# Router scores of nine of twelve token tiles on VectorE instead of TensorE, in a two-layer mixture-of-experts kernel

## The chip, the cores and the metric

The kernel runs on one NeuronCore of a Trainium2 chip. The metric is the device time of one execution in microseconds (us), the median of several runs. The engines are named as in the profile: PE is TensorE, DVE is VectorE, ACT is ScalarE, POOL is GpSimd, SP only issues transfers.

## What is computed

The reference has three parts that follow one another. A recurrent attention over 2 batches, 8 heads and 768 steps gives x of shape (1536, 320). The first mixture (moe) sends every token through all four experts. The second (moe2) sends each token to the one expert with the highest score, out of eight, in slots of limited number:

```python
# first mixture, x: (1536, 320), w1: (4, 320, 1024), w2: (4, 1024, 320)
for e in range(4):
    h = np.maximum(x @ w1[e], 0.0)
    out += p[:, e:e + 1] * (h @ w2[e])
# second mixture, on that out: 8 experts, capacity 384
logits = x @ w_gate                      # w_gate: (320, 8)
expert_idx = np.argmax(logits, axis=1)
gate_w = softmax(logits)[arange(N), expert_idx]
# a token gets the next free slot of its expert; one that finds none is dropped
out[i] = gate_w[i] * y[expert_idx[i], pos[i]]
```

## The kernel before

The 1536 tokens are 12 tiles of 128 tokens, in 4 blocks of 3 tiles (`NT` = 3, `BLOCK` = 384, `BLOCKS1` = 4, `LAST1` = 3). A token's row of 320 features lies in one partition of `acc`, which sums the first mixture's output. Products are made in fp32r with each operand split into a high and a low part, and three products of parts stand for one.

**The loop over experts and blocks.** For each expert e of the first mixture and each block c, PE runs `up` (lines 516 to 531) and `down` (533 to 547). `up` makes 8 tiles of hidden features, f = 0 to 7, each out of 8 matmuls of 384 columns into one of three PSUM banks (`ps_h[f % 3]`). After each one ACT writes `h_hi` (`hidden_hi`, line 795) and then DVE `h_lo` (`hidden_lo`, line 1203). `up` waits ahead of tile f for `h_lo` of tile f - 3, since they share a bank. `down` makes the three token tiles n = 0, 1, 2, each out of 24 matmuls of 320 columns. Within n = 0 it waits ahead of each f for `h_lo` of that f. DVE then adds each tile into `acc` (`add_y`, line 1212). All of it is in program order on each engine. One block of one expert is called a block below, and T0 is the time of its first matmul.

**Weights.** Beside this the next expert's weights are prepared, one piece per block: ACT writes the high parts (`w_to_hi`, lines 787 and 790), DVE the tail (`w_tail`, line 1168, after `hidden_lo` of f = 3), and then POOL the low parts in two instructions (`w1_to_lo`, line 911, after `w_tail`, and `w2_to_lo`, line 919, after ACT's second). POOL's `w_to_lo` of moe2's first expert is needed only when moe2 begins.

**Routing.** The tokens' outputs are final in the last expert's blocks (e = 3). Their routing runs one block behind: in block c (1 to 3) the tiles of block c - 1 are routed, as group c - 1. The last block's tiles are routed as groups 3 (two tiles) and 4 (one tile), partly behind the loop. For a tile of an earlier block PE turns the 128x320 of `acc` with three transposes (`transpose_y`, line 587), ahead of f = 1, 2 and 3. ACT copies the result from PSUM into `yT` (lines 818 and 819), and PE multiplies it with the router's weights, three products of 8 columns (`logits`, line 598), ahead of f = 2, 3 and 4. DVE then chooses the expert (`choose_expert`, lines 1238 to 1253, ahead of and behind `hidden_lo` of f = 5), ACT takes the exponent behind its eight `hidden_hi` (line 824), and PE counts the earlier tokens of each expert (`count_earlier`, lines 603 to 615), ahead of `down`'s tile n = 1. DVE works out gates and slots behind `add_y` of n = 0 (`gates_of`, `slots_of`, lines 1256 to 1276). POOL scatters the group's rows into the table of slots (`scatter_rows`, line 1011) and doubles the last 64 features of each new tile (`repeat_tail`, line 1018).

**The chain on DVE.** Each routing instruction goes through `route`, which increments `route_step` and waits for it, so they follow one another without overlap. `count_earlier` waits for the fifth of a group (`CHOSEN`), and the scatter and the next group's `logits` for the fourteenth (`SLOTS`).

**The end of the loop.** Behind it come the last two groups, 34 products that keep PE busy while the table is read back, and the second mixture, expert by expert, with the same `up` and a `down` of its own (lines 660 to 704), `send` by POOL (line 1036) and w_tail with a share of w2's low part (line 1172).

Of the kernel before, what the change touches and what calls it, by code (L numbers as in the profile page):

```python
# [29 lines left out]
F32 = mybir.dt.float32  # L30
# [8 lines left out]
P = 128  # L39


def build_kernel(nc, gates, o_tok, qk_pair_t, q_t, kv_tok, probs, w_moe1, w_moe2, w_gate, out, capacity):
    BH, S = gates.shape[1:]
    CHUNKS = S // P
    HEADS, D = 8, q_t.shape[1] // 3
# [43 lines left out]
    LAST1 = BLOCKS1 - 1  # L89

    LAST_X = (1, 4)

    WARM_SHORT, WARM_GAP, WARM_LONG = 44, 14, 34

# [9 lines left out]
    with ExitStack() as ctx:  # L104
# [3 lines left out]
        def sem(name):  # L108
            return ctx.enter_context(nc.semaphore(name))
# [73 lines left out]
        w2_lo.append(sb("w2_lo_odd", [P, FT, X], F32R))  # L183
        small = ExitStack()
        empty_row = sb("empty_row", [P, ROW], F32, small)
        yT = [sb(f"yT{i}", [P, KT, P], F32, small) for i in range(NT)]
        top = sb("top", [P, NT], F32, small)
        shifted = sb("shifted", [P, NT, E2], F32, small)
# [105 lines left out]
        yt_psum = sem("yt_psum")  # L294
        yt_done = sem("yt_done")
        log_ready = sem("log_ready")
        route_step = sem("route_step")
        route_exp = sem("route_exp")
        count_ready = sem("count_ready")
# [14 lines left out]
        def _(sp):  # L314
# [48 lines left out]
            for p in range(PIECES):  # L363
                sp.wait_ge(w_ready, p + 1)
                load_piece(w_moe1, 1, p)

            sp.wait_ge(row_const, 1)
            sp.dma_start(table.rearrange("(n p) r -> p n r", p=P),
                         empty_row[:].unsqueeze(1).broadcast_to([P, E2 * NT, ROW])).then_inc(fill_done, 16)
            for par in range(2):  # L370
# [32 lines left out]
        def _(pe):  # L403
# [170 lines left out]
            def transpose_y(t):  # L574

                c, n = t // NT, t % NT
                pe.wait_ge(y_free, 3 + 3 * (G1 - BLOCKS1) + t + 1)
                if c < LAST1:

                    if t:  # L580
                        pe.wait_ge(yt_done, t)
                    dst = ps_yt[0]
                else:
                    dst = ps_yt[n]
                for k in range(KT):
                    width = P if k < 2 else TAIL
                    mm = pe.transpose(dst[0:width, k * P:(k + 1) * P], acc[:, t, k * P:k * P + width], ident[:])
                mm.then_inc(yt_psum, 1)

            def logits(t):  # L590
                for group in range(1, LAST1 + 1):
                    if t == GROUPS[group][0]:

                        pe.wait_ge(route_step, SLOTS * group)
                pe.wait_ge(yt_done, t + 1)
                for k in range(KT):
                    K = P if k < 2 else TAIL
                    mm = pe.matmul(ps_log(t, t + 1)[:, 0, :], yT[t % NT][0:K, k, :], wg[0:K, k, :],  # L598
                                   start=(k == 0), stop=(k == KT - 1))
                if any(t == tiles[-1] for tiles in GROUPS):  # L600
                    mm.then_inc(log_ready, 1)
# [16 lines left out]
            for c in range(BLOCKS1):  # L618
                def before_tile(f):
                    if f % 2 == 0:  # L620
                        pe.wait_ge(w_ready, 4 * e + f // 2 + 1)
                    if c and 2 <= f <= NT + 1:
                        logits(NT * (c - 1) + f - 2)
                    if c and 1 <= f <= NT:
                        transpose_y(NT * (c - 1) + f - 1)

                def before_products(n, f):
                    if c and n == 1 and f == 0:
                        count_earlier(c - 1)
                    if c == LAST1 and n == 2:  # L630
                        if f == 0:
                            transpose_y(TILES - 3)
                        if f == 2:
                            transpose_y(TILES - 2)
                        if f in (3, 4):
                            logits(TILES - 6 + f)
                up(BLOCKS1 * e + c, e % 2, lambda k: xt_hi[:, k, c * BLOCK:(c + 1) * BLOCK],
                   lambda k: xt_lo[:, k, c * BLOCK:(c + 1) * BLOCK], before_tile)
                down(BLOCKS1 * e + c, e % 2, before_products)
# [87 lines left out]
        def _(act):  # L727
# [85 lines left out]
            first_to_hi(3)  # L813

            def yt_to_sbuf(t):
                act.wait_ge(yt_psum, t + 1)
                src = ps_yt[t % NT if t // NT == LAST1 else 0]
                act.activation(yT[t % NT][:, 0:2, :], src[:, 0:2 * P].rearrange("p (k t) -> p k t", k=2), ACT.Copy)
                act.activation(yT[t % NT][0:TAIL, 2, :], src[0:TAIL, 2 * P:XD], ACT.Copy).then_inc(yt_done, 1)

# [20 lines left out]
            for c in range(BLOCKS1):  # L841
                for f in range(FT):
                    hidden_hi(BLOCKS1 * e + c, f)
                    if c and f < NT:
                        yt_to_sbuf(NT * (c - 1) + f)
                    if f in (3, 5):
                        w_to_hi(e + 1, (e + 1) % 2, c, f // 4)
                if c:
                    exp_logits(c - 1)
# [201 lines left out]
        def _(dve):  # L1051
# [184 lines left out]
            def choose_expert(group, part):  # L1236

                n = len(GROUPS[group])
                t = slice(GROUPS[group][0], GROUPS[group][0] + n)
                if part == 0:  # L1240
                    dve.wait_ge(log_ready, group + 1)
                    route(dve.tensor_reduce(top[:, 0:n], ps_log(t.start, t.stop), AX_X, ALU.max))

                    if group:
                        dve.wait_ge(route_exp, group)
                    route(dve.tensor_tensor(shifted[:, 0:n], ps_log(t.start, t.stop), over_e(top[:, 0:n]), ALU.subtract))
                    assert done[0] == SLOTS * group + SHIFTED
                else:
                    route(dve.scalar_tensor_tensor(cand[:, 0:n], shifted[:, 0:n], 0.0, below[:, 0:n],
                                                   ALU.is_equal, ALU.mult))  # L1250
                    route(dve.tensor_reduce(first[:, 0:n], cand[:, 0:n], AX_X, ALU.min))
                    route(dve.tensor_tensor(one_hot[:, t, :], below[:, 0:n], over_e(first[:, 0:n]), ALU.is_equal))
                    assert done[0] == SLOTS * group + CHOSEN
# [33 lines left out]
                return t.unsqueeze(2).broadcast_to([P, t.shape[1], E2])  # L1287


            dve.wait_ge(row_const, 4)  # L1290
            e = E1 - 1
            for c in range(BLOCKS1):
                g = BLOCKS1 * e + c
                for f in range(FT):
                    hidden_lo(g, f)
                    if f == 3:
                        w_tail(e + 1, (e + 1) % 2, c, slice(c * PF, (c + 1) * PF))
                    if c and f in (4, 5):
                        choose_expert(c - 1, f - 4)
                for n in range(NT):  # L1300
                    if c == LAST1 and n == 2:
                        choose_expert(LAST1, 0)
                        choose_expert(LAST1, 1)
                    add_y(g, NT * c + n, n, prob[:, NT * c + n, e:e + 1])
                    if c and n == 0:
                        gates_of(c - 1)
                        slots_of(c - 1)
            gates_of(LAST1)
# [113 lines left out]
```

## Time and profile before

| | us |
|---|---|
| median of 3 runs (each) | 612.3 (614.8, 607.52, 612.3) |
| the profiled execution's own time | 617.45 |
| its span, first to last instruction | 615.4 |
| PE busy | 586.8 |
| DVE busy | 286.2 |
| ACT busy | 217.0 |
| POOL busy | 202.7 |

The span is what the rows below count from; the execution's own time has 2.05 us around it. Busy time counts neither waits nor the issuing of transfers. The mean granted clock of PE over the span is 0.977 of full speed. The profile has several views: the page with its totals, groups of instructions by line, the timeline of one engine (each row: start in us, duration in us, engine, line, operation, output and inputs with shapes, count, and in brackets the idle time before it with what ended it), and windows, a table of each engine's busy time in stretches of time, with PE's granted clock.

### The profile page before, as it was taken

The numbers are of one execution on the slowest core, as the hardware profiler recorded it, in microseconds if no ns is written. First come the engines' busy times: TensorE is split into PE (matmuls) and PEld (weight loads), VectorE is DVE, ScalarE is ACT, GpSimd is POOL, SyncE is SP. The second block draws the span as 40 slices with busy tenths as digits, with TensorE's granted clock in tenths as the row PEclk, the third lists the DMA queues.
The fourth block names the chain that finished last, engine by engine and source line by source line (L and its number), as shares of the span: only waits on it lengthen the run. The fifth ranks groups of instructions, "written<-read, shape, count | busy, mean of one in ns | idle before, by whom it ended". The sixth has DMA issues, their size and how long they took to land.

```text
span 615.4 us, 10948 instructions
## 1 busy us (share of the span) xinstructions
PE 586.8 (95%) x4005; PEld 577.5 (94%) x4005; DVE 286.2 (47%) x597; ACT 217.0 (35%) x475; POOL 202.7 (33%) x226
## 2 busy tenths in 40 slices
PE   3989999999999999999999999999988998899996
PEld 3889989999999999999999999999978998899996
DVE  8577984322332332332233233342434499855472
ACT  5444573312321331232133123132205386546341
POOL 6445548101101110110111021312321567764461
PEclk9888999999999999999999999999987999899999
DMA  6674626931101101110110110211223657764400
GB/s 198 166 218 141 188 91 208 367 145 47 44 3 48 47 0 47 47 35 12 47 47 0 47 48 1 88 48 39 66 81 106 226 160 247 246 221 138 153 16 16
DMA packets 22428, 62.99 MB, mean 102 GB/s; under 512 B 3190, under 2 KB 12543, under 8 KB 22396
## 3 DMA queue, kind: packets, MB, share of 16 engines
q1 hardware_dynamic: 20476, 58.49, 29.5%
q0 software_dynamic: 1920, 4.07, 1.8%
q8 instruction: 21, 0.34, 0.2%
q14 instruction: 11, 0.09, 0.1%
HBM read 51.67 MB, written 13.11 MB: 105 GB/s over the span
## 4 chain that ended last, share of the span: by engine, by line
PE 84%; DVE 4%; DMA 4%; ACT 3%; issue 2%; POOL 1%; POOLq 0%; SPq 0%; DVEq 0%; ACTq 0%
PE bank L528 27%; PE bank L543 9%; PE bank L544 9%; PE bank L545 9%; PE bank L531 4%; PE bank L530 4%; PE bank L685 3%; PE bank L686 3%; PE bank L684 3%; PE bank L492 3%; PE bank L461 2%; DMA g_rows<-g_saved_rows 2%; PE bank L446 1%; PE bank L598 1%; PE bank L482 1%
## 5 line engine op out<-in xcount | busy, mean ns | idle before, releaser
L795 ACT ACTIVATE h_hi<-bank 128x384 fp32r<-128x384 f32 x192 | 94.7, 493 | 312.9 <-PE bank L531 312.8
L1203 DVE SCALAR_TENSOR_TENSOR h_lo<-bank,h_hi 128x384 fp32r<-128x384 f32 x192 | 105.6, 556 | 132.0 <-ACT h_hi L795 131.3
L911 POOL TENSOR_TENSOR w_lo_odd<-stage,w_hi_odd 128x512 fp32r<-128x512 f32 x24 | 31.3, 1303 | 149.2 <-DVE w_hi_odd L1168 119.7
L911 POOL TENSOR_TENSOR w_lo_even<-stage,w_hi_even 128x512 fp32r<-128x512 f32 x24 | 31.3, 1306 | 132.7 <-DVE w_hi_even L1168 119.6
L528 PE MATMUL bank<-xt_hi,w_hi_even 128*128 (+2 forms) x192 | 65.3, 340 | 3.8 <-DVE h_lo L1203 2.1
L528 PE MATMUL bank<-xt_hi,w_hi_odd 128*128 128x384 f32 (+2 forms) x192 | 63.6, 331 | 2.2 <-DVE h_lo L1203 2.2
L1212 DVE SCALAR_TENSOR_TENSOR acc<-bank,prob,acc 128x320 f32 (+1 forms) x36 | 19.8, 551 | 95.8 <-PE bank L545 95.8
L528 PE MATMUL bank<-xt_lo,w_hi_even 128*128 (+2 forms) x192 | 63.6, 331 | 0.0
L528 PE MATMUL bank<-xt_hi,w_lo_even 128*128 (+2 forms) x192 | 63.5, 331 | 0.0
L528 PE MATMUL bank<-xt_lo,w_hi_odd 128*128 128x384 f32 (+2 forms) x192 | 61.8, 322 | 0.0
L528 PE MATMUL bank<-xt_hi,w_lo_odd 128*128 128x384 f32 (+2 forms) x192 | 61.8, 322 | 0.0
L543 PE MATMUL bank<-w_hi_odd,h_hi 128*128 128x320 f32 x192 | 59.9, 312 | 0.0
L543 PE MATMUL bank<-w_hi_even,h_hi 128*128 128x320 f32 x192 | 59.4, 309 | 0.2 <-DVE h_lo L1203 0.2
L544 PE MATMUL bank<-w_lo_odd,h_hi 128*128 128x320 f32 x192 | 59.3, 309 | 0.0
L545 PE MATMUL bank<-w_hi_even,h_lo 128*128 128x320 f32 x192 | 59.3, 309 | 0.0
L545 PE MATMUL bank<-w_hi_odd,h_lo 128*128 128x320 f32 x192 | 59.3, 309 | 0.0
L544 PE MATMUL bank<-w_lo_even,h_hi 128*128 128x320 f32 x192 | 59.3, 309 | 0.0
L528 PEld LDWEIGHTS bank<-xt_hi,w_hi_even 128*128 128x128 f32 x192 | 36.8, 192 | 4.8 <-DVE h_lo L1203 2.6
L528 PEld LDWEIGHTS bank<-xt_hi,w_hi_odd 128*128 128x128 f32 x192 | 36.1, 188 | 2.8 <-DVE h_lo L1203 2.7
L528 PEld LDWEIGHTS bank<-xt_lo,w_hi_even 128*128 128x128 f32 x192 | 36.9, 192 | 0.0
L528 PEld LDWEIGHTS bank<-xt_hi,w_lo_even 128*128 128x128 f32 x192 | 36.7, 191 | 0.0
L755 ACT ACTIVATE dmat<-bank,cols 128x128 f32<-128x128 f32 x96 | 27.2, 366 | 27.0 <-PE bank L446 27.0
(183 smaller groups left out, 1348.4 us busy)
## 6 DMA issues: line engine op xcount, KB each, us to landing
stage<-w_moe SPq DMA_DIRECT2D x48, 704.0 KB, 4.1
slot_rows<-empty_row SPq DMA_DIRECT2D x1, 4632.0 KB, 20.1
x_slot<-slot_rows SPq DMA_DIRECT2D x24, 193.0 KB, 4.3
kv<-kv_tok SPq DMA_DIRECT2D x12, 324.0 KB
qk_pair<-qk_pair_t SPq DMA_DIRECT2D x24, 160.0 KB
q_rows<-q_t SPq DMA_DIRECT2D x12, 180.0 KB
sig<-o_tok SPq DMA_DIRECT2D x2, 960.0 KB, 6.5
out<-empty_row SPq DMA_DIRECT2D x2, 960.0 KB, 17.8
```

Of the source, the lines that this page charges most:

```text
L492: mm = pe.matmul(ps_in[:, h * V1:(h + 1) * V1], pmat[:, h, :], v41[j][:, h, :], start=True, stop=True)
L528: pe.matmul(dst, wk[w][:, k, cols], xk(k), start=(n == 0), stop=False)
L530: pe.matmul(dst, w1_hi[w][:, 2, cols], xh(2), start=False, stop=False)
L531: pe.matmul(dst, w1_hi[w][:, 2, cols], xl(2), start=False, stop=True).then_inc(h_psum, 1)
L543: pe.matmul(ps_y[n][:, 0:X], h_hi[:, f, rows], w2_hi[w][:, f, :], start=(f == 0), stop=False)
L544: pe.matmul(ps_y[n][:, 0:X], h_hi[:, f, rows], w2_lo[w][:, f, :], start=False, stop=False)
L545: mm = pe.matmul(ps_y[n][:, 0:X], h_lo[:, f, rows], w2_hi[w][:, f, :], start=False, stop=(f == FT - 1))
L755: op = act.activation(dmat[b][:, h, :], src[:, n * P:(n + 1) * P], ACT.Exp, bias=cols3[:, c, b * HEADS + h:b * HEADS + h + 1])
L795: act.activation(h_hi[:, f, :], ps_h[f % 3][:, 0:BLOCK], ACT.Relu).then_inc(h_hi_done, 1)
L911: return pool.tensor_tensor(w1_lo[w][:, :, cols], raw1[:, 0:2, :], w1_hi[w][:, 0:2, cols].bitcast(F32), ALU.subtract)
L1203: dve.scalar_tensor_tensor(h_lo[:, f, :], ps_h[f % 3][:, 0:BLOCK], 0.0, h_hi[:, f, :].bitcast(F32), ALU.max, ALU.subtract).then_inc(h_done, 1)
L1212: op = dve.scalar_tensor_tensor(acc[:, tile, 0:X], ps_y[n][:, 0:X], share, acc[:, tile, 0:X], ALU.mult, ALU.add)
```

## The change

The scores of groups 0 to 2 (nine tiles) are made on DVE. The router's weights come in a second array, `w_gate_rows` (8 x 320), which is sent to all 128 partitions with one broadcast transfer. One score of 128 tokens is one `scalar_tensor_tensor`, (acc * 1.0) * weights' row, with the sum in `accum_out`: 24 of them to a group. Two stand behind each `hidden_lo` of a block and eight behind the last one. Then comes `choose_expert`. PE's `transpose_y` and `logits` and ACT's copies of `yT` for these groups are left out, `count_earlier` moves from n = 1 to n = 2 of `down`, and gates and slots from behind `add_y` of n = 0 to behind that of n = 1. The tiles of the last block go as before.

```diff
+        wg_rows = sb("wg_rows", [P, E2, X], F32, small)
+        products = [sb(f"products{i}", [P, X], F32, small) for i in range(3)]
+        logit = sb("logit", [P, TILES - NT, E2], F32, small)
...
             sp.wait_ge(row_const, 1)
+            sp.dma_start(wg_rows[:], w_gate_rows.unsqueeze(0).broadcast_to([P, E2, X])).then_inc(wg_rows_in, 16)
             sp.dma_start(table.rearrange("(n p) r -> p n r", p=P),
...
                 def before_tile(f):
                     if f % 2 == 0:
                         pe.wait_ge(w_ready, 4 * e + f // 2 + 1)
-                    if c and 2 <= f <= NT + 1:
-                        logits(NT * (c - 1) + f - 2)
-                    if c and 1 <= f <= NT:
-                        transpose_y(NT * (c - 1) + f - 1)
 
                 def before_products(n, f):
-                    if c and n == 1 and f == 0:
+                    if c and n == 2 and f == 0:
                         count_earlier(c - 1)
...
                     hidden_hi(BLOCKS1 * e + c, f)
-                    if c and f < NT:
-                        yt_to_sbuf(NT * (c - 1) + f)
...
                 if part == 0:
-                    dve.wait_ge(log_ready, group + 1)
-                    route(dve.tensor_reduce(top[:, 0:n], ps_log(t.start, t.stop), AX_X, ALU.max))
+                    if group < LAST1:
+                        dve.wait_ge(dot_done, NT * E2 * (group + 1))
+                        log = logit[:, t, :]
+                    else:
+                        dve.wait_ge(log_ready, group - LAST1 + 1)
+                        log = ps_log(t.start, t.stop)
+                    route(dve.tensor_reduce(top[:, 0:n], log, AX_X, ALU.max))
...
+            def dots(group, part):
+                for n in range(DOTS * part, DOTS * (part + 1)):
+                    t = NT * group + n // E2
+                    if n % E2 == 0:
+                        dve.wait_ge(y_free, 3 + 3 * (G1 - BLOCKS1) + t + 1)
+                    k = NT * E2 * group + n
+                    if k >= 3:
+                        dve.wait_ge(dot_done, k - 2)
+                    dve.scalar_tensor_tensor(products[k % 3][:], acc[:, t, 0:X], 1.0, wg_rows[:, n % E2, :], ALU.mult, ALU.mult,
+                                             accum_out=logit[:, t, n % E2:n % E2 + 1]).then_inc(dot_done, 1)
...
             dve.wait_ge(row_const, 4)
+            dve.wait_ge(wg_rows_in, 16)
...
                     if f == 3:
                         w_tail(e + 1, (e + 1) % 2, c, slice(c * PF, (c + 1) * PF))
-                    if c and f in (4, 5):
-                        choose_expert(c - 1, f - 4)
+                    if c:
+                        dots(c - 1, f)
+                if c:
+                    for part in range(FT, NT * E2 // DOTS):
+                        dots(c - 1, part)
+                    choose_expert(c - 1, 0)
+                    choose_expert(c - 1, 1)
                 for n in range(NT):
                     if c == LAST1 and n == 2:
                         choose_expert(LAST1, 0)
                         choose_expert(LAST1, 1)
                     add_y(g, NT * c + n, n, prob[:, NT * c + n, e:e + 1])
-                    if c and n == 0:
+                    if c and n == 1:
                         gates_of(c - 1)
                         slots_of(c - 1)
```

`DOTS` is 2 and `E2` is 8. The new tiles lie in the memory that later holds the slots' rows.

## Rows read from the trace of the kernel before

**Rows 1.** The page, part 1: busy time, share of the span, instructions.

```profile
PE 586.8 (95%) x4005; PEld 577.5 (94%) x4005; DVE 286.2 (47%) x597; ACT 217.0 (35%) x475; POOL 202.7 (33%) x226
```

**Rows 2.** Windows, last expert's blocks 0 and 1: length, engines' busy, clock, DMA share, GB/s.

```profile
349.36:371.01 21.65, 21.65 (x139) 21.65 (x137) 6.53 (x12) 5.29 (x10) 3.35 (x4) 1.00 0.11 34
371.01:396.31 25.30, 25.30 (x168) 25.04 (x167) 9.81 (x26) 6.90 (x17) 6.23 (x6) 1.00 0.14 46
```

**Rows 3.** Timeline of PE, block 1 of the last expert.

```profile
371.01 0.33 PE L528 MATMUL bank<-xt_hi,w_hi_odd 128*128 128x384 f32 x1
...
374.12 0.82 PE L598 MATMUL bank<-wg,yT 128*128 128x8 f32 x6
...
381.42 0.34 PE L528 MATMUL bank<-xt_hi,w_hi_odd 128*128 128x384 f32 x1
...
385.58 0.31 PE L543 MATMUL bank<-w_hi_odd,h_hi 128*128 128x320 f32 x1
```

**Rows 4.** Timeline of DVE, the same block.

```profile
373.12 0.56 DVE L1203 SCALAR_TENSOR_TENSOR h_lo<-bank,h_hi 128x384 fp32r<-128x384 f32 x1 [1.35 <-ACT h_hi L795]
...
384.28 0.18 DVE L1251 TENSOR_REDUCE first<-cand 128x3 f32<-128x24 f32 x1
384.50 1.32 DVE L1252 TENSOR_TENSOR one_hot<-below,first 128x24 bf16<-128x24 f32 x1
385.85 1.02 DVE L1203 SCALAR_TENSOR_TENSOR h_lo<-bank,h_hi 128x384 fp32r<-128x384 f32 x2
```

**Rows 5.** Timeline of POOL, the same block.

```profile
381.13 1.29 POOL L911 TENSOR_TENSOR w_lo_even<-stage,w_hi_even 128x512 fp32r<-128x512 f32 x1 [9.07 <-DVE w_hi_even L1168]
384.20 1.57 POOL L919 TENSOR_TENSOR w_lo_even<-stage,w_hi_even 128x640 fp32r<-128x640 f32 x1 [1.78 <-ACT w_hi_even L790]
392.58 1.19 POOL L1011 DMA_INDIRECT slot_rows<-acc,slot  x1 [6.80 <-DVE slot L1275]
...
396.33 0.42 POOL L1018 COPY acc<-acc 128x64 f32<-128x64 f32 x2
```

**Rows 6.** Timeline of DVE, second mixture: operations on SBUF alone, and what follows them.

```profile
475.78 0.49 DVE L1172 TENSOR_TENSOR w_lo_odd<-stage,w_hi_odd 128x320 fp32r<-128x320 f32 x1
476.19 0.55 DVE L1203 SCALAR_TENSOR_TENSOR h_lo<-bank,h_hi 128x384 fp32r<-128x384 f32 x1
...
481.44 0.18 DVE L1334 COPY gate_s<-x_slot 128x3 f32<-128x3 f32 x1
481.54 0.15 DVE L1335 CAST token_s<-x_slot 128x3 uint32<-128x3 f32 x1
```

**Rows 7.** One line's instructions, durations in ns: minimum, median, maximum.

```profile
L1249 DVE SCALAR_TENSOR_TENSOR cand<-shifted,below x5: 167/173/175, 384.1 to 453.0; 128x24 f32<-128x24 f32 x3, 128x16 f32<-128x16 f32 x1, 128x8 f32<-128x8 f32 x1
```

**Rows 8.** Timeline of ACT, block 1 of the last expert.

```profile
383.39 0.73 ACT L790 ACTIVATE w_hi_even<-stage 128x640 fp32r<-128x640 f32 x1
```

**Rows 9.** Timelines of DVE, POOL and PE in the second mixture.

```profile
509.25 2.98 DVE L1172 TENSOR_TENSOR w_lo_odd<-stage,w_hi_odd 128x320 fp32r<-128x320 f32 x1
...
509.75 1.31 POOL L911 TENSOR_TENSOR w_lo_odd<-stage,w_hi_odd 128x512 fp32r<-128x512 f32 x1
511.00 0.87 POOL L919 TENSOR_TENSOR w_lo_odd<-stage,w_hi_odd 128x320 fp32r<-128x320 f32 x1
...
512.75 0.38 PE L528 MATMUL bank<-xt_hi,w_hi_even 128*128 128x256 f32 x1 [2.07 <-DVE h_lo L1203]
...
527.37 0.39 PE L528 MATMUL bank<-xt_hi,w_hi_odd 128*128 128x256 f32 x1 [2.18 <-DVE h_lo L1203]
```

**Rows 10.** Windows of 1 us behind the two gaps; the column before the last two is the clock.

```profile
514.00:515.00 1.00, 1.00 (x9) 1.00 (x8) 0.99 (x2) 1.00 (x3) 0.44 (x1) 1.00 0.89 366
...
529.00:530.00 1.00, 1.00 (x6) 1.00 (x5) 0.99 (x3) 1.00 (x3) 0.13 (x2) 0.50 0.77 321
...
532.00:533.00 1.00, 1.00 (x9) 1.00 (x8) 0.96 (x4) 0.00 (x0) 0.01 (x1) 0.96 0.28 93
```

**Rows 11.** The page, part 5: ACT's copies of the staged weights.

```profile
L787 ACT ACTIVATE w_hi_even<-stage 128x768 fp32r<-128x768 f32 x24 | 20.4, 849 | 0.0
```

More of the change, by code:

```diff
@@ L39, with build_kernel @@
 P = 128
-def build_kernel(nc, gates, o_tok, qk_pair_t, q_t, kv_tok, probs, w_moe1, w_moe2, w_gate, out, capacity):
+def build_kernel(nc, gates, o_tok, qk_pair_t, q_t, kv_tok, probs, w_moe1, w_moe2, w_gate, w_gate_rows, out, capacity):
     BH, S = gates.shape[1:]
@@ L91, in build_kernel @@
     LAST_X = (1, 4)
+    DOTS = 2
     WARM_SHORT, WARM_GAP, WARM_LONG = 44, 14, 34
@@ L296, in build_kernel @@
         log_ready = sem("log_ready")
+        wg_rows_in = sem("wg_rows_in")
+        dot_done = sem("dot_done")
         route_step = sem("route_step")
@@ L577, in transpose_y @@
                 pe.wait_ge(y_free, 3 + 3 * (G1 - BLOCKS1) + t + 1)
[L578 to L584, printed above, removed]
+                dst = ps_yt[n]
                 for k in range(KT):
@@ L590, in logits @@
             def logits(t):
[L591 to L595, printed above, removed]
+                if t == GROUPS[LAST1][0]:
+                    pe.wait_ge(route_step, SLOTS * LAST1)
+                pe.wait_ge(yt_done, t - NT * LAST1 + 1)
                 for k in range(KT):
@@ L815, in yt_to_sbuf @@
             def yt_to_sbuf(t):
-                act.wait_ge(yt_psum, t + 1)
-                src = ps_yt[t % NT if t // NT == LAST1 else 0]
+                act.wait_ge(yt_psum, t - NT * LAST1 + 1)
+                src = ps_yt[t % NT]
                 act.activation(yT[t % NT][:, 0:2, :], src[:, 0:2 * P].rearrange("p (k t) -> p k t", k=2), ACT.Copy)
@@ L1240, in choose_expert @@
                 if part == 0:
-                    dve.wait_ge(log_ready, group + 1)
-                    route(dve.tensor_reduce(top[:, 0:n], ps_log(t.start, t.stop), AX_X, ALU.max))
+                    if group < LAST1:
[5 more added lines that the diff above has]
+                    route(dve.tensor_reduce(top[:, 0:n], log, AX_X, ALU.max))
                     if group:
                         dve.wait_ge(route_exp, group)
-                    route(dve.tensor_tensor(shifted[:, 0:n], ps_log(t.start, t.stop), over_e(top[:, 0:n]), ALU.subtract))
+                    route(dve.tensor_tensor(shifted[:, 0:n], log, over_e(top[:, 0:n]), ALU.subtract))
                     assert done[0] == SLOTS * group + SHIFTED
@@ L1412 @@
         "w_gate": w_gate,
+        "w_gate_rows": inputs["moe2_w_gate"].T,
     }
```

## The prediction

> **What bounds the kernel now.** The page's totals come first: PE is busy 95% of the span, DVE 47% [rows 1]. The chain that ended last runs over PE's matmuls almost throughout, so time taken from PE's program counts in full, as long as its feeders keep pace. Next, the windows of the stretch in question: a block without routing takes 21.65 us and the next, with routing, 25.30 us, PE being busy throughout at full clock [rows 2]. DVE is busy 6.53 and 9.81 us in them, so it seems to have 15 us to spare. But the reader has to see when that time is free. DVE's h_lo is what PE waits for: PE's tile f needs h_lo of f - 3, and the product f of the first token tile needs h_lo of f. Work put between them is on the path once it outgrows its gap.
>
> **What goes.** Between T0 = 371.01 and 381.42 PE makes five hidden tiles, and three more up to 385.58, 1.387 us each [rows 3]. Five would take 6.93 us; they took 10.41. So nine transposes and eighteen small products cost 3.48 us a block, 10.4 us in three blocks. ACT's copies go too; ACT has room already, so this is worth nothing by itself. One group of each kind of row shows it: the products L598 at 374.12 stand between hidden tiles with nothing beside them [rows 3].
>
> **What one dot costs.** No row shows an instruction with `accum_out`. The nearest is DVE's 128x320 operation with two inputs in SBUF: 0.49 us long, the next one starting 0.41 us behind it [rows 6]. Then the sum has to be written. At best that is hidden: 0.41 us. At worst it waits for the end of the main part and takes a small chained routing operation's step, 0.22 us from 384.28 to 384.50 [rows 4]: 0.49 + 0.20 = 0.69. A small operation that waits for nothing costs 0.10 us (481.44 to 481.54) [rows 6]. I take 0.58, which is 0.49 and about that 0.10. It is nearest to what a second small instruction should cost behind one whose end it needs.
>
> The Trainium skill (VectorE: DVE Perf Modes, "Two Vector instructions with no wait between them") says that an operation which also writes its accumulator is two instructions. It gives no price; the ends above stand without it.
>
> A wait stands ahead of each dot, for the dot three before it. That has long ended, so it costs nothing. Behind it queue the next h_lo, and PE for that.
>
> **Where they fall: the up phase.** Times are from T0. The first h_lo starts at 2.11 and the spacing of two is 0.46 to 0.47 [rows 4]. ACT offers a new one each 1.387 us. An h_lo and two dots take 0.47 + 1.16 = 1.63, so DVE falls behind from the start: h_lo of f = 1, 2, 3 at 3.74, 5.37 and 7.00. w_tail then ends at about 8.0.
>
> Now a second thing. POOL makes its two low parts, 1.29 and 1.57 us [rows 5], and while it does so, DVE's operations with both inputs in SBUF stand. In this very block one_hot, a 0.17 us operation by its neighbours, starts at 384.50 and takes 1.32 us, to 385.82, just behind POOL's end at 384.20 + 1.57 = 385.77 [rows 4, 5]. A w2 part in the second mixture took 2.98 us in place of 0.49, over two POOL instructions that follow each other directly (509.75 to 511.87) [rows 9]. h_lo reads PSUM and SBUF and isn't held; a dot is. POOL starts as w_tail ends, one dot passes, and the second one stands. ACT's second part has ended by 9.7 (it is 0.73 us long and follows hidden tile 5) [rows 8], so POOL's second instruction follows the first at once, to about 11.35. That dot ends at 11.8, and h_lo of f = 4, queued behind it, at 12.4. PE needs it for tile 7, due at 9.71: a stall of 2.75 us. Tile 7 ends at 13.84. h_lo of 5, 6, 7 start at 13.43, 15.06, 16.69; the last ends at 17.25. PE wants it at 16.92, and 0.35 us more go. Tiles n = 0 and 1 of down end at 17.74 and 21.26 (3.52 each, from 10.56 us a down in the plain block [rows 2, 3]).
>
> **The down phase.** DVE has ten dots left from 17.16, so it is at 22.96. Then come the drain of the last (0.1) and five chained routing operations of 0.21: CHOSEN at 24.1. `count_earlier` waits for that, and PE's tile n = 2 is queued behind it: a wait of 2.85 us, though the change moved the count a whole tile later. Tile 2 ends at 27.8 (0.1 for the count, then 3.52). The block takes 27.8 us against 25.3: +2.5, or +7.5 for three. DVE then has its adds, gates and slots (13 short operations, some 3 us) done by 27, so nothing is carried over to the next T0.
>
> **Edges.** POOL's scatter starts some 5 us later in the block than now (21.6), at about 27, and takes 3.75 us up to the copies (392.58 to 396.33) [rows 5]. So three copies of 0.24 fall into the next block's first dots and hold them: 0.5 us, in two blocks, +1.0. In block 3 the transposes of the new tile wait for `add_y` behind CHOSEN (0.3), and its scores for the slots of group 2 at 27 (0.5): +0.8. The broadcast transfer of 1.3 MB on SP's queue stands ahead of the table's filling in the first expert. It delays the weights of the third by some us, but ACT's copies of them show no idle time at all ahead of them [rows 11], so it costs nothing.
>
> **The clock.** PE's waits of 2.85 us are new. The trace has two waits of nearly this size: behind one of 2.07 us the granted clock stayed at 1.00, the 2.4 GHz level; behind one of 2.18 us it fell to 0.50, the 1.2 GHz level, from 529 to just past 532 [rows 9, 10]. Three us at half speed cost 1.6. The new waits are longer than both. The wait in the up phase lies ahead of PE's longer wait in down, which absorbs a slower n = 0 and 1; the wait ahead of n = 2 isn't covered by anything. I count two falls of three: +3.2, with 0 and 4.8 as ends.
>
> **Sum.** 7.5 + 1.0 + 0.8 + 3.2 = 12.5 us. The profiled execution's own 617.45 becomes 629.95. It lies 5.15 over the median shown, 612.3, and on that scale the forecast is 624.8, slower by 2.0%.
>
> **Rivals.**
> 1. *The two sides cancel.* With a dot at 0.50 or less, each block is shorter by 24 x 0.08 = 1.9 us or more, which leaves +0.6 or less a block, and the waits of PE drop under 1.5 us, below the one that left the clock alone. With the edges the sum is between -1 and +4: 611 to 616. For it: the spacing of 0.41 [rows 6]. Against: the sum must be written. The bound to the forecast lies at 0.52.
> 2. *Faster.* POOL's lows hold no dot, and a dot takes 0.48 or less. Then h_lo of 7 ends by 12.7 (2.11 + 7 x 1.43 + 0.56), PE's up phase keeps its 11.1, and CHOSEN comes at 19.1, 1 us behind n = 1: the block takes 22.8, -2.5 each, 605. The decisive point is the hold; [rows 4, 5] and [rows 9] both speak for it, so this is unlikely.
> 3. *The dot runs at half rate.* 320 elements cost 0.33 us more, 0.91 in all; DVE bounds the block by 24 x 0.33 = 7.9 us more, +24 in three blocks: 648. Against it: the same kind of instruction with two SBUF inputs takes 0.167 us at 8 elements and 0.173 at 24 [rows 7]. At half rate 16 elements more should cost 0.033. These are short operations, though, and carry no sum.
>
> The Trainium skill (Vector Engine (DVE) Microarchitecture Reference, "Points that are easy to get wrong") says of this instruction that two SBUF sources which aren't bf16 halve its throughput, as no port is left for the accumulator. That is rival 3. By that rule the time would be the 648 above; the trace so far leans against it.
>
> **How the numbers follow.** About 1% (6 us) is what a measurement of this kernel can tell from no change. Chances: the forecast and its neighbourhood (dot 0.52 to 0.69) 0.54, rival 1 0.24, rival 2 0.10, rival 3 0.12. Faster by over 1%: 0.10. Within: 0.24. Slower: 0.66. The forecast's own range is from 618 (dot 0.52) to 0.11 x 24 x 3 = 8 us over it with a third fall of the clock, 635. With rival 1 at the lower end and something of a dearer dot at the upper one the range is 608 to 640; it leaves out most of rivals 2 and 3.
>
> **What would show it.** In the changed profile: dots of 0.49 us with a second small row or a gap behind each, spacing 0.58; in each of three blocks one dot of 2 us or more beside POOL's L911 and L919; PE waiting for h_lo at tile 7 and for one_hot ahead of n = 2, both 2 to 3 us; PE's rows L587 and L598 down to a quarter; windows of 27 to 29 us per block, some with the clock under 1.00. If those windows are under 25.3, DVE's slack was real and the forecast is wrong; if dots beside POOL keep their length, the hold is the step that failed; if the blocks exceed 33, it is the price of a dot.

## The result, and the profile after

The median of 20 runs is 609.4 us against 613.2 us of 20 runs before. The ratio is 0.9945, with a 95% interval of 0.9919 to 0.997: faster by 0.3 to 0.8%, some 2 to 5 us. Here and below, ratios and intervals leave out runs over 1.5% above the fastest of their kernel. The forecast was slower by 12.5 us, so the sign is wrong. The profiled execution has a span of 609.2 us against 615.4, but half of that difference means nothing for the change. Block 1 begins at 367.86 in place of 371.01 [rows 3], so 3.15 us were gained ahead of the altered blocks. That is how one execution differs from another: over the profiles of all runs below the same T0 lies anywhere from 364.2 to 375.7. The one thing altered ahead of it is the broadcast transfer, and ACT's first copies of the staged weights have one and the same wait for a transfer in both kernels, 2.6 us near 100 us (ahead of a copy into w_hi_odd, which the row of [rows 11] leaves out), so it cost nothing, as predicted. The blocks have to be compared from their own T0.

Windows of the changed kernel: the last expert's blocks 0, 1 and 3 (the columns are those of [rows 2]).

```profile
346.21:367.86 21.65, 21.65 (x139) 21.65 (x137) 6.54 (x12) 5.29 (x10) 3.35 (x4) 1.00 0.11 34
367.86:391.98 24.12, 22.51 (x142) 21.70 (x140) 20.84 (x74) 5.51 (x11) 3.45 (x4) 1.00 0.10 32
...
416.16:441.00 24.84, 23.06 (x151) 21.84 (x149) 20.85 (x74) 6.59 (x15) 7.37 (x9) 1.00 0.16 54
```

Block 0 is unaltered at 21.65. Block 1 takes 24.12 us in place of 25.30 [rows 2], block 2 24.18 in place of 25.39, and from the last T0 to the second mixture's first matmul it is 42.39 in place of 43.30. That is 1.18 + 1.21 + 0.91 = 3.3 us, close to the medians' 3.8. DVE is busy 20.84 of 24.12 us, where it was 9.81 of 25.30, and PE now has 1.6 us of idle time. The clock stays at 1.00.

Timeline of DVE, block 1 of the changed kernel. L1198 is `hidden_lo`, L1299 the dot.

```profile
370.44 0.48 DVE L1299 SCALAR_TENSOR_TENSOR products<-acc,wg_rows 128x320 f32<-128x320 f32 x1
370.85 0.08 DVE L1299 DVE_READ_ACCUMULATOR products<-acc,wg_rows 128x1 f32 x1
370.85 0.48 DVE L1299 SCALAR_TENSOR_TENSOR products<-acc,wg_rows 128x320 f32<-128x320 f32 x1
...
375.31 0.49 DVE L1299 SCALAR_TENSOR_TENSOR products<-acc,wg_rows 128x320 f32<-128x320 f32 x1
375.73 0.08 DVE L1299 DVE_READ_ACCUMULATOR products<-acc,wg_rows 128x1 f32 x1
375.73 1.58 DVE L1299 SCALAR_TENSOR_TENSOR products<-acc,wg_rows 128x320 f32<-128x320 f32 x1
377.24 0.08 DVE L1299 DVE_READ_ACCUMULATOR products<-acc,wg_rows 128x1 f32 x1
377.24 0.55 DVE L1198 SCALAR_TENSOR_TENSOR h_lo<-bank,h_hi 128x384 fp32r<-128x384 f32 x1
377.71 1.77 DVE L1299 SCALAR_TENSOR_TENSOR products<-acc,wg_rows 128x320 f32<-128x320 f32 x1
...
387.96 0.18 DVE L1252 TENSOR_TENSOR one_hot<-below,first 128x24 bf16<-128x24 f32 x1
```

The first three rows are the whole surprise. A dot is indeed two instructions, but the one that writes the sum starts at the same 370.85 as the next dot. It begins in the last 0.07 us of the main part and takes next to no time of its own: the spacing is 0.41 us. The next rows show the hold that was forecast, but in another form: two of the block's dots take 1.58 and 1.77 us, and an h_lo gets in between them. The forecast had one dot stand through both of POOL's instructions.

Timeline of POOL in the same block, and PE's waits in it.

```profile
375.36 1.59 POOL L906 TENSOR_TENSOR w_lo_even<-stage,w_hi_even 128x512 fp32r<-128x512 f32 x1 [6.45 <-DVE w_hi_even L1163]
377.57 1.56 POOL L914 TENSOR_TENSOR w_lo_even<-stage,w_hi_even 128x640 fp32r<-128x640 f32 x1 [0.61 <-ACT w_hi_even L787]
```

```profile
383.01 0.41 PE L551 MATMUL bank<-w_hi_odd,h_hi 128*128 128x320 f32 x1 [0.43 <-DVE h_lo L1198]
...
388.29 0.17 PE L608 MATMUL bank<-one_hot,tri 128*128 128x24 bf16 x1 [1.06 <-DVE one_hot L1252]
```

POOL's first instruction is 0.3 us longer than in [rows 5]: a dot began just ahead of it, at 375.31, and the same excess stands beside a dot in the other runs (1.58 to 1.61), while without one it takes 1.28 to 1.30. The second dot, at 375.73, then ends at 377.31, 0.36 behind POOL's end at 376.95. POOL's second instruction starts 0.61 us later, as it waits for ACT's copy, and in that gap h_lo of f = 4 starts. It ends at 377.79, and PE starts hidden tile 7 at 377.84:

```profile
377.84 0.44 PE L536 MATMUL bank<-xt_hi,w_hi_odd 128*128 128x384 f32 x1
```

That is 0.27 us behind its due time of T0 + 9.71, too little for the profile to show a wait, where 2.75 were forecast. PE waits 0.43 us for the last h_lo of `down`'s n = 0, and 1.06 us for CHOSEN, which is done at 388.14, 20.28 behind T0.

### The profile page after: what moved, and what is told of

It is laid out like the page before. It is cut to its first block, busy times and chain, and to the rows that moved or that the text cites. A ratio compares the mean times of both kernels' runs of the same rounds, so it can differ in the third digit from the quotient of the medians.

```text
span 609.2 us, 10906 instructions
## 1 busy us (share of the span) xinstructions
PE 577.8 (95%) x3924; PEld 566.5 (93%) x3924; DVE 318.7 (52%) x741; ACT 213.0 (35%) x457; POOL 204.2 (34%) x226
## 4 chain that ended last, share of the span: by engine, by line
PE 79%; DVE 10%; ACT 3%; DMA 3%; issue 2%; POOL 2%; POOLq 0%; SPq 0%; DVEq 0%; ACTq 0%
PE bank L536 26%; PE bank L551 8%; PE bank L553 8%; PE bank L552 8%; DVE products L1299 5%; PE bank L539 4%; PE bank L538 4%; PE bank L683 3%; PE bank L682 3%; PE bank L500 3%; PE bank L681 3%; PE bank L469 2%; PE bank L454 1%; PE bank L482 1%; DVE h_lo L1198 1%
## 5 line engine op out<-in xcount | busy, mean ns | idle before, releaser
L1198 DVE SCALAR_TENSOR_TENSOR h_lo<-bank,h_hi 128x384 fp32r<-128x384 f32 x192 | 105.8, 556 | 111.5 <-ACT h_hi L792 110.6
L906 POOL TENSOR_TENSOR w_lo_even<-stage,w_hi_even 128x512 fp32r<-128x512 f32 x24 | 32.2, 1344 | 118.0 <-DVE w_hi_even L1163 104.8
L1299 DVE SCALAR_TENSOR_TENSOR products<-acc,wg_rows 128x320 f32<-128x320 f32 x72 | 38.6, 582 | 0.1
L551 PEld LDWEIGHTS bank<-w_hi_odd,h_hi 128*128 128x128 f32 x192 | 36.1, 188 | 2.1 <-DVE h_lo L1198 2.1
## 6 DMA issues: line engine op xcount, KB each, us to landing
slot_rows<-empty_row SPq DMA_DIRECT2D x1, 4632.0 KB, 22.8
```

Source lines behind the costliest of these rows:

```text
L551: pe.matmul(ps_y[n][:, 0:X], h_hi[:, f, rows], w2_hi[w][:, f, :], start=(f == 0), stop=False)
L906: return pool.tensor_tensor(w1_lo[w][:, :, cols], raw1[:, 0:2, :], w1_hi[w][:, 0:2, cols].bitcast(F32), ALU.subtract)
L1198: dve.scalar_tensor_tensor(h_lo[:, f, :], ps_h[f % 3][:, 0:BLOCK], 0.0, h_hi[:, f, :].bitcast(F32), ALU.max, ALU.subtract).then_inc(h_done, 1)
L1299: dve.scalar_tensor_tensor(products[k % 3][:], acc[:, t, 0:X], 1.0, wg_rows[:, n % E2, :], ALU.mult, ALU.mult, accum_out=logit[:, t, n % E ...
```

## The experiments

Two theories stood after the result. A: only the price of a dot was wrong; DVE's chain up to CHOSEN, POOL's hold on it and PE's waits are as worked out. B, in several forms: the other terms were smaller too, so that the block's length is set by something else. Line numbers of a variant may be shifted by a few lines. Blocks are measured from T0 to the next T0, of blocks 1 and 2. The medians come from different rounds: the kernel before had 611.84 in those of x1, x3, x4 and x5, 611.83 in those of x2, x6, x7 and x8, and 612.7 (one run) in those of x9 and x10.

| run | CHOSEN behind T0 (block 1) | blocks 1 and 2 | median, us |
|---|---|---|---|
| before | - | 25.30, 25.39 | 613.2 (20 runs) |
| changed | 20.28 | 24.12, 24.18 | 609.4 (20) |
| x5, dot at 0.58 | 23.82 | 29.17, 29.33 | 623.95 (4) |
| x3, dots twice | 29.66 | 35.03, 34.93 | 646.7 (1) |
| x4, twice, second plain | 29.41 | 35.75, 34.85 | 641.24 (1) |
| x2, count ahead of n = 1 | 20.28 | 29.60, 30.16 | 628.68 (4) |
| x9, three dots | 19.88 | 25.39, 26.44 | 622.5 (1) |
| x10, one dot | 21.07 | 26.28, 26.52 | 616.85 (1) |
| x7, before with late lows | - | 25.30, 25.39 | 613.84 (10) |
| x1, changed with late lows | 17.90 | 21.83, 21.89 | 605.21 (7) |
| x8, changed again | 20.28 | 24.10, 24.20 | 609.66 (12) |
| x6, late lows again | 17.90 | 21.82, 21.90 | 604.64 (12) |

**The dot at the predicted price.** A short product is put behind each dot.

```diff
...
+                    dve.scalar_tensor_tensor(spare[k % 3][:, 0:96], acc[:, t, 0:96], 1.0, wg_rows[:, n % E2, 0:96],
+                                             ALU.mult, ALU.mult).then_inc(spare_done, 1)
```

> The changed kernel, with a second, 96 columns wide product behind each dot, so that a dot and its companion cost 0.41 + 0.17 = 0.58 us, the price of the prediction. If that price was the only wrong term (A), blocks 1 and 2 take 27.5 to 28.3 us, with PE waits of 2.5 to 3 us at hidden tile 7 and ahead of n = 2, and the kernel is 11 us slower than the changed one with the clock untouched and up to 16 with falls of the clock: ratio to before 1.012 to 1.02. If other terms of the prediction were wrong as well (B: the hold or the waits are smaller than worked out), a block stays under 26.5 us and the ratio under 1.005.

Timeline of PE in blocks 1 and 2 of this run, at its long waits only, and two windows: block 1, and four us right behind block 1's second wait.

```profile
376.56 0.44 PE L539 MATMUL bank<-xt_hi,w_hi_odd 128*128 128x384 f32 x1 [2.36 <-DVE h_lo L1201]
...
388.30 0.17 PE L611 MATMUL bank<-one_hot,tri 128*128 128x24 bf16 x1 [2.63 <-DVE one_hot L1255]
...
405.80 0.69 PE L539 MATMUL bank<-xt_hi,w_hi_odd 128*128 128x384 f32 x1 [2.42 <-DVE h_lo L1201]
...
417.54 0.17 PE L611 MATMUL bank<-one_hot,tri 128*128 128x24 bf16 x1 [1.67 <-DVE one_hot L1255]
```

```profile
364.33:393.50 29.17, 24.02 (x141) 23.21 (x140) 24.58 (x98) 5.52 (x11) 4.99 (x5) 0.94 0.08 26
...
388.00:392.00 4.00, 3.71 (x17) 3.74 (x18) 2.66 (x12) 0.00 (x0) 0.08 (x1) 0.57 0.00 0
```

Both waits of the prediction are there, at the places named: in block 1 2.36 us for 2.75 and 2.63 for 2.85. CHOSEN is at 23.82 for the predicted 24.1. The clock falls behind the second wait. From CHOSEN to the block's end it takes 5.35 us, 3.84 in the changed kernel, so the fall costs 1.5 and the block is 29.17. In block 2 the clock falls already at the end of the wait of 2.42 (0.50 from 405.4 to 408.6) and again 1.5 us behind that of 1.67. The second wait is shorter there, as the slower matmuls ahead of it use up part of it: this is the absorption that the prediction argued. The prediction counted two falls in three blocks; this execution has four (block 3 has one, behind a wait of 2.36).

From T0 of block 1 to the second mixture's first matmul it is 104.8 us, 94.0 in the kernel before: slower by 10.8, where 12.5 were forecast. The four runs are 617.44, 620.32, 627.59 and 629.38. By the first two the ratio is 1.012 (618.88 against 611.84 in the same rounds), at the lower end of the 1.012 to 1.020 expected and with too few runs for an interval; it doesn't show the forecast's 2%. What the run shows is the course within the blocks: with the price of 0.58 DVE's chain, the places of PE's waits and the block's length (27.8 and a fall of the clock) are as the prediction worked them out, and the blocks are far over the 26.5 of theory B. Theory A holds for them. One thing differs: no instruction stands through both of POOL's. The first companion takes 1.35 us, then a dot passes in 0.48, and the next companion takes 1.57.

**Each dot twice, with and without a second sum.**

```diff
...
+                    dve.scalar_tensor_tensor(spare[k % 3][:, 0:X], acc[:, t, 0:X], 1.0, wg_rows[:, n % E2, 0:X],
+                                             ALU.mult, ALU.mult, accum_out=spare_sum[k % 3][:]).then_inc(spare_done, 1)
```

> The changed kernel, each dot followed by a second one with a sum of its own into spare memory: 48 a block. A (0.41 us for main part and sum together, DVE bounds the block): blocks 1 and 2 at 24.1 + 24 x 0.41 = 33.9 us, +0.5 at most for a PE clock that falls in the waits. If the sum's writing overlaps only where the next instruction is something else (B), spacing of two dots is 0.49 or more and a block is over 35.8.

> As the run with each dot twice, but the second product of each pair writes no sum. A (the sum costs nothing): spacing 0.41 and blocks within 0.3 us of that run's, 33.9. B (the sum's writing costs its own 0.07 to 0.08 us somewhere): a block shorter by 24 x 0.08 = 1.9 us.

Timeline of DVE with two sums (first fence: L1302 and L1306 both write one), and with one (second fence: L1302 writes a sum, L1306 doesn't).

```profile
370.50 0.49 DVE L1306 SCALAR_TENSOR_TENSOR spare<-acc,wg_rows 128x320 f32<-128x320 f32 x1
370.91 0.08 DVE L1306 DVE_READ_ACCUMULATOR spare<-acc,wg_rows 128x1 f32 x1
370.91 0.49 DVE L1302 SCALAR_TENSOR_TENSOR products<-acc,wg_rows 128x320 f32<-128x320 f32 x1
```

```profile
369.86 0.49 DVE L1306 SCALAR_TENSOR_TENSOR spare<-acc,wg_rows 128x320 f32<-128x320 f32 x1
370.26 0.48 DVE L1302 SCALAR_TENSOR_TENSOR products<-acc,wg_rows 128x320 f32<-128x320 f32 x1
```

The spacing is 0.41 with a sum and 0.40 without, and CHOSEN differs by 0.25 us over 24 sums: 0.01 us for each. A sum's own 0.08 would have made 1.9. CHOSEN moved by 9.38 and 9.13 us for 24 instructions more, where 24 x 0.41 = 9.84 was expected. Most of the difference is idle time: in the changed kernel DVE stands still for 0.09 us ahead of each of three h_lo and 0.18 ahead of w_tail, and the added dots fill that. The blocks, 35.03 and 35.75, were over the 33.9 to 34.4 expected and lie in the wrong order, because the clock fell around PE's waits of 3.37 and 4.1 to 5.1 us and not equally in the two. The reader should take CHOSEN, which DVE alone sets, and not the block. The times of these two runs stand on one execution each.

**POOL's low parts later**, so that they hold no dot.

```diff
             for c in range(BLOCKS1):
+                if c:
+                    pool.wait_ge(route_step, SLOTS * (c - 1) + CHOSEN)
                 w_to_lo(E1, E1 % 2, c)
```

> The changed kernel, with POOL's two low parts of a block (L911 and L919 of before) made behind the choice of experts in place of behind w_tail. Theory A (a dot costs 0.41 us, and POOL's two instructions hold DVE for 1.1 + 1.3 us a block): no dot is longer than 0.6 us, CHOSEN comes 2.4 us earlier, PE's waits ahead of n = 0's last product (0.43) and of n = 2 (1.06) go, and a block takes 21.9 to 22.3 us in place of 24.1. Against the changed kernel -6 us, against the kernel before about -9.5 (ratio 0.984). Rival B (the hold only moves, to the adds, gates and slots, and the later scatter is late at the end of the loop): a block of 23 us or more, the loop's end not over 2 us earlier than in the changed kernel, ratio 0.991 or more.

Windows of its block 1, and all its dots, durations in ns as minimum, median and maximum.

```profile
367.71:389.54 21.83, 21.83 (x142) 21.73 (x141) 19.22 (x74) 5.51 (x11) 3.07 (x3) 1.00 0.01 2
```

```profile
L1301 DVE SCALAR_TENSOR_TENSOR products<-acc,wg_rows x72: 475/492/574, 370.3 to 427.8; 128x320 f32<-128x320 f32 x72
```

No dot is longer than 0.574 us, where the changed kernel has up to 1.77. CHOSEN comes 2.38 us earlier, PE's waits in the block are gone, and the block is 21.83, which is 0.18 over a block without any routing. The hold itself hasn't gone: it now falls on an operation of `slots_of`, 0.87 us in place of 0.18, for which PE doesn't wait.

```profile
387.70 0.87 DVE L1274 TENSOR_TENSOR spot<-spot,over 128x24 f32<-128x24 f32 x1
```

From T0 of block 1 to the second mixture's first matmul it is 84.6 us, 90.7 in the changed kernel and 94.0 before. The time did not show all of that at first: a ratio to before of 0.9911 (0.9879 to 0.9942), where 0.984 was expected. So it was run again, beside the changed kernel in the same rounds.

> The changed kernel unaltered, as the partner of the next run in the same rounds. Blocks 1 and 2 at 24.1 us; ratio to before 0.992 to 0.997, as first measured.

> The kernel with POOL's low parts behind the choice of experts once more. Its first profile had blocks of 21.83 and 21.89 us, and the second mixture began 6.1 us earlier in it, counted from the same T0, than in the changed kernel; its ratio to before was 0.991 (0.988 to 0.994) all the same, where -9.5 us would be 0.984. Theory A (the gain of 6 us is real and the scatter of single runs, through PE's clock, hid part of it): this time's median is 4 to 7 us under that of the changed kernel. Rival B (about 3 us are given back in some executions, in the second mixture or at the loop's end): 2 to 3.5 us under it again, with profiles whose distance from T0 to the second mixture's first matmul is the same 84.6 us and whose rest is longer than 147 us.

The medians of 12 runs each are 609.66 and 604.64 us: 5.0 us apart, within the 4 to 7 of theory A. The ratios to before are 0.9971 (0.9929 to 1.0013) and 0.9896 (0.9858 to 0.9935). The interval of the changed kernel includes no change this time; that it is faster rests on the first 20 runs and on the blocks. The blocks repeat to 0.02 us: 24.10 and 24.20, 21.82 and 21.90. The repeated profile has 86.5 us from T0 to the second mixture and not 84.6, with the same blocks. It is of an execution of 609.27 us, over the median of its own kernel, and the clock falls at other places of the loop's end in it (0.50 from 438.8 to 442 and from 445.3 to 448.6, in the first profile once, from 439.9 to 446.4). Whether that makes the 1.9 us, and how often it happens, is open. The variant with late low parts beats both kernels, by about 1% against the one before.

**The same edit on the kernel before.**

> The kernel before, with POOL's low parts behind the choice of experts as in the other run: nothing else of the change. Theory A (the hold costs only where DVE is late): one_hot falls from 1.32 to 0.18 us, blocks stay at 25.3 us, time the same within 0.3%. Rival (late low parts are worth something by themselves): blocks shorter by 0.5 us or more.

Windows of block 1, and one_hot in it.

```profile
368.17:393.47 25.30, 25.30 (x168) 25.04 (x167) 8.76 (x26) 6.91 (x17) 6.19 (x6) 1.00 0.13 46
```

```profile
381.65 0.18 DVE L1254 TENSOR_TENSOR one_hot<-below,first 128x24 bf16<-128x24 f32 x1
```

one_hot takes 0.18 us in place of 1.32 [rows 4], and the block is 25.30 in both: a hold on an engine with slack costs nothing. The ratio came out at 1.0056 (1.0012 to 1.0099), slower than the blocks explain. That misses the 0.3% expected. The distance from T0 to the second mixture is 93.7 against 94.0, so whatever it is lies elsewhere or is scatter; it wasn't followed up.

**The count back in its old place.**

```diff
-                    if c and n == 2 and f == 0:
+                    if c and n == 1 and f == 0:
                         count_earlier(c - 1)
```

> The changed kernel with the count of earlier tokens back in front of n = 1 of down. Theory A (CHOSEN, 20.3 us behind T0, is what PE waits for): the wait now stands 7.04 us of products ahead of the block's end in place of 3.52, blocks 1 and 2 take 27.5 us, PE waits 4 to 4.6 us there, and the kernel is 10 to 13 us slower than the changed one: ratio to before 1.010 to 1.018. Rival (the move of the count is worth little, since h_lo holds PE as well): blocks under 25.5 us, ratio under 1.002.

Timeline of PE at the count, and the window right behind it.

```profile
394.38 0.18 PE L608 MATMUL bank<-one_hot,tri 128*128 128x24 bf16 x1 [4.58 <-DVE one_hot L1252]
```

```profile
394.38:398.00 3.62, 3.62 (x16) 3.62 (x17) 0.44 (x1) 0.00 (x0) 0.00 (x0) 0.50 0.00 0
```

PE waits 4.58 us for the same CHOSEN at 20.28, and then runs at the 1.2 GHz level, so that the block is 29.60 in place of the 27.5 expected: the clock, which the expectation left out, makes the other 2 us. The ratio is 1.0217 (1.0125 to 1.0309), by two of the four runs, over the 1.010 to 1.018 expected. Without the move of the count the change would have lost more than it gained.

**How the dots are spread.** One edit each, `DOTS = 3` and `DOTS = 1`.

> The changed kernel with three dots behind each hidden_lo and none behind the last. DVE's sum up to CHOSEN is the same, 20.3 us behind T0, but h_lo comes later. Theory A by the same working as before, with 0.41 a dot: PE waits about 2.5 us at hidden tile 7 and 0.6 us at n = 0's last product, n = 1 ends at 21.3, behind CHOSEN, so the wait ahead of n = 2 is gone and a block takes 24.9 us. Rival (only CHOSEN counts): a block of 24.1 us.

> The changed kernel with one dot behind each hidden_lo and sixteen behind the last. Theory A (CHOSEN sets the block's length, and DVE's sum up to it is the same): no wait for h_lo, PE waits 1.5 to 2.1 us ahead of n = 2, a block still takes 24.0 to 24.2 us. Rival (the waits for h_lo cost their own part): a block shorter by 0.4 us, 23.7.

Timeline of PE with three dots, its wait in block 1 and in block 2, and a window behind the latter.

```profile
388.25 0.45 PE L536 MATMUL bank<-xt_hi,w_hi_odd 128*128 128x384 f32 x1 [2.65 <-DVE h_lo L1198]
...
413.71 0.44 PE L536 MATMUL bank<-xt_hi,w_hi_odd 128*128 128x384 f32 x1 [2.72 <-DVE h_lo L1198]
```

```profile
414.00:416.00 2.00, 2.00 (x8) 2.00 (x8) 2.00 (x10) 0.00 (x0) 0.00 (x0) 0.53 0.85 284
```

Three dots gave the waits as worked out, 2.65 us at hidden tile 7, 0.37 at n = 0's last product, and none ahead of n = 2; block 1 is 25.39 for the expected 24.9, and block 2, with a fall of the clock, 26.44. CHOSEN is even earlier than with two dots, 19.88, and the block is longer all the same, so CHOSEN isn't the only thing that counts. One dot missed its expectation of a wait of 1.5 to 2.1 us and a block of 24.0 to 24.2. DVE now has gaps, and its chain to CHOSEN is longer by 0.8 us (first fence DVE, second PE):

```profile
367.71 0.56 DVE L1198 SCALAR_TENSOR_TENSOR h_lo<-bank,h_hi 128x384 fp32r<-128x384 f32 x1 [0.42 <-ACT h_hi L792]
```

```profile
385.44 0.18 PE L608 MATMUL bank<-one_hot,tri 128*128 128x24 bf16 x1 [2.93 <-DVE one_hot L1252]
```

It waits 0.42 us for ACT ahead of three h_lo in a row, where a second dot would have left 0.09. The fourth h_lo starts at the same 6.27 behind T0 as with two dots, but three dots fewer are done by then, 1.23 us; 0.46 comes back, as an h_lo, which isn't held, lies beside POOL's first instruction (the dot behind it takes 1.12 in place of 1.58). CHOSEN comes at 21.07, PE waits 2.93 us, and the clock falls around that in each block (0.50 from 386 to 388 in block 1). From CHOSEN to the block's end it takes 5.21, so 1.4 of the 26.28 are the clock's. So the sum of DVE's work isn't the same whatever the order: dots in a gap are free, dots moved out of it aren't. Both runs have one execution each.

## Why the prediction was wrong

**What bounds the kernel, and what goes.** Right. Once DVE is out of PE's way, the block is 21.83 us, so the transposes and products were worth the 3.48 us they were priced at.

**What one dot costs.** This is the step that failed: "I take 0.58". The runs show 0.41, the lower end of its own bounds, of which 0.01 is the sum's. The two instructions that the Trainium skill (VectorE: DVE Perf Modes, "Two Vector instructions with no wait between them") names are both in the trace as rows of their own; the mistake was to let the second one cost issue time behind the end of the first. [rows 6] had half of the answer. The operation of 0.49 us is followed after 0.41, so its last 0.08 us lie beside the next one; even with the 0.10 of a small operation added, that makes 0.51 and not 0.58. That the second instruction takes almost nothing no row of before shows. A step "whose end it needs" was assumed, not read. 24 x 0.17 = 4.1 us a block is what the wrong price adds before anything else follows from it.

**The up phase.** DVE as what PE waits for was right, and so was the hold as such; its form wasn't. The prediction took from the 2.98 us of [rows 9] that one dot stands through both of POOL's instructions. In no run does one: a held instruction gets in between the two, in the changed kernel through a gap of 0.61 us in which POOL waits for ACT, and in the run with each dot twice also where POOL's second follows at once (dots of 1.57 and 1.80). What the hold takes in all, 1.1 and 1.3 us, is close to what was worked out, and CHOSEN pays 2.38 of it; but h_lo of 4 lies between the two parts, at 9.38 in the changed kernel, and so the wait of 2.75 at hidden tile 7 was 0.27. With a dot of 0.41 and the hold in two parts the same working puts h_lo of 5 at about 12.0 and CHOSEN at 20.3; the changed kernel has 11.96 and 20.28. The spacing of 1.29 is then shorter than ACT's 1.387, so DVE no longer falls behind by itself, only through the hold. In time the hold costs the 5 us between x8 and x6.

**The down phase.** CHOSEN was rightly what PE waits for ahead of n = 2. The wait is 1.06 us in place of 2.85.

**The clock.** It was counted with two falls in three blocks, 3.2 us. None came in the changed kernel's blocks, where no wait is over 1.06 us. Elsewhere the length of a wait decides less than the prediction hoped. Around waits of 2.72, 2.93 and 4.58 us the clock fell to 0.50, and behind one of 2.65 it stayed. In x5 it stayed behind waits of 2.36 and 1.50, and fell at or behind others of 2.36, 2.42, 2.63 and even 1.67 us. A fall cost 1.0 to 2.0 us of its block; in x5's block 2, where a later wait took up most of the loss, the second fall made the block only 0.16 longer.

**Edges.** The loop's third part gave 0.91 where the other two gave 1.2, so the edges cost 0.3 and not the 1.8 predicted. POOL's three copies do fall into the next block's first dots, as forecast, but they hold them by 0.1 us and not 0.5; it is POOL that takes longer, 1.15 us for the three, where one alone takes 0.24.

```profile
395.89 1.15 POOL L1013 COPY acc<-acc 128x64 f32<-128x64 f32 x3
```

```profile
395.95 0.55 DVE L1299 SCALAR_TENSOR_TENSOR products<-acc,wg_rows 128x320 f32<-128x320 f32 x1
```

**Rivals.** The true course was the one between rivals 1 and 2. Rival 1 had the right mechanism, but its sum of -1 to +4 belongs to a dot of about 0.44 to 0.50 (worked back from the sum), though the row that speaks for it says 0.41. At 0.41 its own working gives 27.8 - 4.1 = 23.7 us a block, faster by 1.6 each. That the median of 609.4 lies inside the stated 608 to 640 is owed to rival 1, which the range took in, and not to the forecast. Rival 2's block of 22.8 needed the hold gone; the run with late low parts, where it is gone, reached 21.83. Rival 3 is refuted: the dot is 0.48 us long, no longer than [rows 6]'s operation of the same shape without a sum. The Trainium skill (Vector Engine (DVE) Microarchitecture Reference, "Points that are easy to get wrong") says that this instruction runs at half rate with two SBUF sources that aren't bf16. The trace disagrees, at 0.48 us for 320 elements of fp32, and decides.

## What to carry to other kernels

Price an instruction on a busy in-order engine by the spacing from its start to the next one's start, not by its duration, and a second small instruction behind it by the same reading; where a bound is wide, work out the sum at both ends, since a queue that just keeps pace turns a 40% dearer instruction into the other sign. Before an engine's slack is spent, look at which other engine's rows lengthen the operations that fill it: here the holds took more than half of what the change could have given, and one wait moved on POOL gave it back. What work added to an engine costs is read at the instructions that others wait for, here CHOSEN and, with three dots in a row, h_lo of f = 4; moving CHOSEN's consumer later was worth more than the whole net gain.

## What the runs showed of the hardware

The instruction that writes a VectorE accumulator has its own row of 71 to 84 ns and takes 0.01 us of the engine's time: it starts together with the next main part. A VectorE operation with two inputs in SBUF is held while GpSimd subtracts tiles in SBUF (dots of 1.58 and 1.77 us in place of 0.48), and GpSimd in turn takes 0.3 us longer beside such an operation that began first (1.59 us in place of 1.29). An operation that reads PSUM and SBUF isn't held: in x10 an h_lo from 372.09 takes 0.55 us inside POOL's first instruction (371.72 to 373.33). The size of the held operation makes no difference in these runs: the companion of 96 columns (1.35 us) and one_hot of 24 (1.32 us) were held to GpSimd's end too. GpSimd's short copies of 64 columns held dots by under 0.1 us each (0.55 and 0.51 in place of 0.48). Whether a held operation gets in between two GpSimd instructions that follow each other directly isn't settled: the dots of x3 did (1.57 and 1.80 us), the operation of 2.98 us in [rows 9] didn't.
